# Block products in the last two thirds of an MLP's first layer, and attention tiles moved forward to feed them

## The reference

```python
# q, k, v: [4, 8, 576, 64], chunks of 64 tokens
scores = (q_c @ k_c.T) / 8;  attn = softmax(scores);  out = attn @ v_c
x = out as [2304 tokens, 512]
h = x @ w_in;  g = h - tanh(h);  x = g @ w_out                      # MLP 1, w_in [512, 2048]
h = x @ w2_in; g = h * tanh(softplus(h));  out = g @ w2_out         # MLP 2
```

## Time and profile before

| | |
|---|---|
| median of the runs | 824.29 us |
| time of the profiled execution | 823.91 us |
| its span, first to last instruction | 822.1 us |
| TensorE busy (matmul) | 812.8 us, 99% |
| VectorE busy | 543.9 us, 66% |
| ScalarE busy | 361.9 us, 44% |
| GpSimd busy | 150.5 us, 18% |
| DMA traffic | 132.21 MB, mean 161 GB/s |

### The profile page before, as it was taken

One profiled execution on the slowest core, in us unless ns is written; L12 is line 12 of the kernel. 1 busy time (PEld: TensorE's weight loads), 2 busy tenths in 40 slices (PEclk: granted clock), 3 DMA queues, 4 the chain that ended last, 5 costly groups with the idle time before them and its releaser, 6 DMA issues.

```text
span 822.1 us, 13517 instructions
## 1 busy us (share of the span) xinstructions
PE 812.8 (99%) x5394; PEld 765.6 (93%) x5394; DVE 543.9 (66%) x819; ACT 361.9 (44%) x567; POOL 150.5 (18%) x213
## 2 busy tenths in 40 slices
PE   7999999999999999999999999999999999999998
PEld 6999999999999999999999889888988988888896
DVE  6766555655555655534447788888877777877775
ACT  4544433343344344333335455546445435445434
POOL 4322244334415413410110111110000000000000
PEclk9999999999999999999999999999999999999999
DMA  7653355444425434422654265397424276523302
GB/s 242 210 177 99 101 186 193 133 159 180 168 74 198 157 115 157 179 65 90 231 194 164 90 231 192 129 354 311 153 92 177 90 272 236 195 90 127 143 0 77
DMA packets 41597, 132.21 MB, mean 161 GB/s; under 512 B 7104, under 2 KB 10944, under 8 KB 41536
## 3 DMA queue, kind: packets, MB, share of 16 engines
q1 hardware_dynamic: 29088, 83.38, 28.2%
q0 software_dynamic: 12448, 47.98, 16.6%
HBM read 91.49 MB, written 35.91 MB: 155 GB/s over the span
## 4 chain that ended last, share of the span: by engine, by line
PE 91%; DVE 5%; ACT 2%; issue 1%; DMA 0%; SPq 0%
PE psum L945 8%; PE psum L946 8%; PE psum L944 8%; PE psum L931 8%; PE psum L932 7%; PE psum L933 7%; PE psum L1080 7%; PE psum L1081 7%; PE psum L1079 7%; PE psum L1058 6%; PE psum L1059 6%; PE psum L1057 6%; PE psum L892 1%; PE psum L858 1%; PE psum L978 1%
## 5 line engine op out<-in xcount | busy, mean ns | idle before, releaser
L673 DVE TENSOR_TENSOR pool_words<-psum,pool_words 128x384 f32<-128x384 f32 x96 | 53.4, 557 | 120.3 <-ACT pool_words L466 120.3
L946 PE MATMUL psum<-g_hi,w_lo 128*128 128x384 f32 x384 | 128.4, 334 | 0.0
L945 PE MATMUL psum<-g_lo,w_hi 128*128 128x384 f32 x384 | 128.3, 334 | 0.0
L944 PE MATMUL psum<-g_hi,w_hi 128*128 128x384 f32 x384 | 128.3, 334 | 0.0
L931 PE MATMUL psum<-x_hi,w_hi 128*128 128x384 f32 x360 | 122.2, 340 | 0.7 <-DVE w_lo L606 0.7
L932 PE MATMUL psum<-x_lo,w_hi 128*128 128x384 f32 x360 | 120.4, 334 | 0.0
L933 PE MATMUL psum<-x_hi,w_lo 128*128 128x384 f32 x360 | 120.3, 334 | 0.0
L466 ACT ACTIVATE pool_words<-psum 128x384 f32<-128x384 f32 x96 | 46.9, 489 | 146.3 <-PE psum L933 144.3
L1058 PE MATMUL psum<-w_lo,w_hi 128*128 128x384 f32 x288 | 97.5, 339 | 0.0
L1059 PE MATMUL psum<-w_hi,w_lo 128*128 128x384 f32 x288 | 97.0, 337 | 0.0
L1057 PE MATMUL psum<-w_hi 128*128 128x384 f32 x288 | 96.3, 334 | 0.0
(11 more groups left out here) (110 smaller groups left out, 1532.1 us busy)
## 6 DMA issues: line engine op xcount, KB each, us to landing
w_hi<-s_hi SPq DMA_DIRECT2D x24, 896.0 KB, 4.6
w_lo<-s_lo SPq DMA_DIRECT2D x24, 896.0 KB, 6.8
pool_words<-w_out POOLq DMA_DIRECT2D x32, 256.0 KB, 3.8
w_hi<-t_hi SPq DMA_DIRECT2D x18, 384.0 KB, 4.9
w_lo<-t_lo SPq DMA_DIRECT2D x18, 384.0 KB, 5.6
pool_words<-w POOLq DMA_DIRECT2D x24, 256.0 KB, 3.7
pool_words<-qT SPq DMA_DIRECT2D x18, 256.0 KB, 3.8
pool_words<-kT SPq DMA_DIRECT2D x18, 256.0 KB, 5.1
```

The costliest lines, as they stand in the source:

```text
L944: pe.matmul(ps, w_hi[:, 1, cols], g_hi[:, s, :], start=f == 0, stop=False)
L945: pe.matmul(ps, w_hi[:, 1, cols], g_lo[:, s, :], start=False, stop=False)
L946: mm = pe.matmul(ps, w_lo[:, 1, cols], g_hi[:, s, :], start=False, stop=f == FT - 1)
```

## The change

Groups 0 and 1 of MLP 1 stay plain (`PLAIN = 2`). The other four groups become two supers of 768 tokens, done as MLP 2 is: 16 pairs q = 0 to 15 of seven block products (`product1`, six matmuls of 128x384), six additions each, then tanh, subtraction and the two parts on 768 columns. `y1_wide(u, j)`, the output step, keeps the weights stationary as `y1` does and takes 768 tokens as three matmuls of 512 and three of 256. Eight more sets of weight sums are made (now of `w_in` too), stored and loaded back. The second super's input sums are made in place, without a way through HBM.

The input of the first super is tiles 6 to 11, so all attention tiles up to 11 must be finished in groups 0 and 1: nine blocks stand there instead of six. The other six stand behind the products of pairs 0 to 5 (tiles 12 to 17). The bodies of `order_blocks`, `turn_blocks`, `shift`, `normalise`, `wait_for_values`, `scores`, `values`, `hidden` and `y1` are unchanged, and so is the order within an f of `mlp1_group`. The buffers in `pool_words` are laid out anew.

```diff
+PLAIN = 2
...
+ORDER1 = (M1, M2, M6, M7, M4, M5, M3)
...
+BLOCK_AT = {(0, 5): 3, (0, 8): 4, (0, 11): 5, (0, 14): 6, (1, 1): 7, (1, 4): 8, (1, 7): 9, (1, 9): 10, (1, 11): 11}
+BLOCK_BEHIND = {0: 12, 2: 13, 3: 14, 4: 15, 5: 16, 6: 17}
+STEPS_AFTER = {1: (0, 0, 0, 0, 1, 1, 2), PAIRS + 1: (2, 2, 0, 0, 1, 1, 2)}
+STEPS_BESIDE_PAIR = (2, 0, 2, 0, 2, 1, 1)
+STEPS_BESIDE_BLOCK = (1, 1, 0, 0, 1, 1, 1)
...
+place_steps([("group", 0, f) for f in (12, 13, 14)], weight_steps(0))
+place_steps([("group", 1, f) for f in range(1, 13)], [step for j in range(1, 5) for step in weight_steps(j)])
+place_steps([(1, 1), (1, 2), (1, 3)], _T0[0:3])
+place_steps([(2, 1), (2, 2), (2, 3)], [_T0[3], weight_steps(5)[0], _T0[4]])
+place_steps([(3, 1), (3, 2), (3, 3)], [weight_steps(5)[1], _T0[5], weight_steps(5)[2]])
+place_steps([(4, 0), (4, 1), (4, 2), (4, 3)], [_T0[6]] + weight_steps(6))
+place_steps([(5, 1), (5, 2), (5, 3)], weight_steps(7))
+place_steps([(6, 1), (6, 2), (6, 3)], weight_steps(8))
+place_steps([(PAIRS, 3), (PAIRS + 1, 1), (PAIRS + 1, 2), (PAIRS + 1, 3)], weight_steps(9)[0:2] + [_T1[0], weight_steps(9)[2]])
+for _i in range(1, 7):
+    place_steps([(PAIRS + 1 + _i, r) for r in range(4)], [_T1[_i]] + weight_steps(9 + _i))
+EARLY_STEPS = len(STEPS)
...
+            def add_x(w):
+                b11, b21, b12, b22 = (x_block(w, t, k) for t in range(2) for k in (0, HALF_K))
+                pool.wait_ge(x_next_done, (9, 15)[w])
+                pool.tensor_tensor(b12, b22, b12, ALU.subtract).then_inc(x_sums, 1)
+                pool.wait_ge(x1_lo_done, 7 * w + 1)
+                pool.wait_ge(x_sums, 4 * w + 1)
+                pool.tensor_tensor(b11, b12, b11, ALU.add).then_inc(x_sums, 1)
+                pool.wait_ge(x1_lo_done, 7 * w + 2)
+                pool.wait_ge(x_sums, 4 * w + 2)
+                pool.tensor_tensor(b21, b11, b21, ALU.subtract).then_inc(x_sums, 1)
+                pool.wait_ge(x1_lo_done, 7 * w + 3)
+                pool.wait_ge(x_sums, 4 * w + 3)
+                pool.tensor_tensor(b11, b22, b11, ALU.subtract).then_inc(x_sums, 1)
+            def load_w2_out(v):
+                if v >= 2:
...
+            for t in range(GROUP_TILES, 13):
                 sp.wait_ge(scores_ready, t)
                 load_qk(t)
                 if t > GROUP_TILES:
                     order_blocks(t - 1)
                 sp.wait_ge(values_ready, t)
                 load_v(t)
-            order_blocks(TILES - 1)
-            before = FT * (GROUPS - 1)
-            for pair in range(2):
-                sp.wait_ge(h_ready, before - (-(pair + 1) * 7 * BLOCK // D_MODEL))
-                load_slot(pair)
-            for i in range(7):
-                end = FT if i == M3 else -(-(2 * 7 * BLOCK + (i + 1) * WIDE) // D_MODEL)
-                sp.wait_ge(h_ready, before + end)
-                load_tokens(0, i)
+                if t in (10, 11):
+                    sp.wait_ge(h_ready, FT - (-(t - 9) * 7 * BLOCK // D_MODEL))
+                    load_slot(t - 10)
+            sp.wait_ge(scores_ready, 13)
+            load_qk(13)
+            order_blocks(12)
+            for q in range(PAIRS1):
+                if q == PAIRS1 - 1:
+                    for i in range(7):
+                        sp.wait_ge(product1_ready, 7 * q + i + 1)
+                        load_tokens(0, i)
+                sp.wait_ge(product1_ready, 7 * (q + 1))
+                if q not in BLOCK_BEHIND:
+                    load_slot(q + 2)
+                    continue
+                t = BLOCK_BEHIND[q]
+                sp.wait_ge(values_ready, t + 1)
+                if t + 1 < TILES:
+                    load_v(t + 1)
+                if t + 2 < TILES:
+                    sp.wait_ge(scores_ready, t + 2)
+                    load_qk(t + 2)
+                load_slot(q + 2)
+                if t + 1 < TILES:
+                    order_blocks(t + 1)
...
+            def mlp1_pair(q):
+                if q - 1 in BLOCK_BEHIND and BLOCK_BEHIND[q - 1] + 1 < TILES:
+                    exps(BLOCK_BEHIND[q - 1] + 1)
+                beside_pair_hi(q, 0)
+                keep_m1_1(q)
+                if q == 0:
+                    split_g_hi(PLAIN * FT - 1)
+                    x1_hi(0, 6)
+                if q == 1:
+                    keep_y(1)
+                if q > 0:
+                    hi1(2 * q - 1)
+                beside_pair_hi(q, "w0")
+                if q == PAIRS + 1:
+                    keep_wide_y(0)
+                for r in range(1, 4):
+                    beside_pair_hi(q, r)
+                beside_pair_hi(q, "w1")
+                tanh1(2 * q)
+                hi1(2 * q)
+                tanh1(2 * q + 1)
+                if q in BLOCK_BEHIND:
+                    keep_x(BLOCK_BEHIND[q])
 
             exps(0)
             exps(1)
@@ -534,8 +755,11 @@
...
+            def mlp1_pair(q):
+                scored = BLOCK_BEHIND.get(q - 1, TILES) + 1
+                if scored < TILES:
+                    shift(scored)
+                if q > 0:
+                    minus1(2 * q - 1)
+                beside_pair_lo(q, 0)
+                if q > 0:
+                    lo1(2 * q - 1)
+                take1_c11(q)
+                if q == 0:
+                    split_g_lo(PLAIN * FT - 1)
+                beside_pair_lo(q, "w0")
+                if q == 1:
+                    keep_y(1)
+                take1_u2(q)
+                if q == 0:
+                    x1_lo(0, 6)
+                if scored < TILES:
+                    normalise(scored)
+                beside_pair_lo(q, 1)
+                take1_u3(q)
+                if scored < TILES:
+                    turn_blocks(scored)
+                if q == PAIRS + 1:
+                    keep_wide_y(0)
+                beside_pair_lo(q, 2)
+                take1_c21(q)
+                beside_pair_lo(q, 3)
+                take1_c22(q)
+                beside_pair_lo(q, "w1")
+                minus1(2 * q)
+                take1_c12(q)
+                lo1(2 * q)
 
             shift(0)
             shift(1)
@@ -734,8 +1064,11 @@
             split_chunk_lo(1)
             split_chunk_lo(2)
             minus_tanh(0)
...
+            def product1(q, place):
+                w, r, i = q // PAIRS, q % 2, ORDER1[place]
+                pe.wait_ge(slot_loaded[r], 32 * (q // 2 + 1))
+                if q % PAIRS == 0:
+                    pe.wait_ge(x1_lo_done, 7 * w + place + 1)
...
+                    pe.wait_ge(x_next_done, t - 2)
+                    if t + 1 < TILES:
+                        pe.wait_ge(shifted, t + 2)
+                if q == 0 and place in (2, 3):
+                    pe.wait_ge(g_done, PLAIN * FT - 3 + place)
+                if q == 1 and place < 4:
+                    pe.wait_ge(sums1_taken, (2, 3, 4, 6)[place])
+                if q > 1 and place < 2:
+                    pe.wait_ge(sums1_taken, 6 * (q - 1) + (4, 6)[place])
+                if q > 1 and place == 2 or q == 0 and place == 4:
+                    pe.wait_ge(m1_kept1, q + 1)
+                if q > 1 and place == 3 or q == 0 and place == 5:
+                    pe.wait_ge(sums1_taken, 6 * q + 1)
+                if q > 0 and place in (4, 5):
+                    pe.wait_ge(sums1_taken, 6 * q + place - 2)
+                if place == 6:
+                    pe.wait_ge(sums1_taken, 6 * q + 5)
+                ps = product1_ps(q, place)
+                t_hi_words = token_words(w_hi, x_hi, place).rearrange("p (k n) -> p k n", k=HALF_K)
+                t_lo_words = token_words(w_lo, x_lo, place).rearrange("p (k n) -> p k n", k=HALF_K)
+                for k in range(HALF_K):
+                    first, end = i != M3 and k == 0, i != M5 and k == HALF_K - 1
...
+            def y1_wide(u, j):
+                w, f = u // (UNITS1 // 2), unit_tile(u)
+                start, end = u % (UNITS1 // 2) == 0, u % (UNITS1 // 2) == UNITS1 // 2 - 1
...
+                    pe.wait_ge(lo1_done, u + 1)
+                    if u == 0:
+                        pe.wait_ge(m1_kept1, 2)
+                        pe.wait_ge(sums1_taken, 6 + 1)
+                    if start:
+                        pe.wait_ge(y_kept, (2 * KT, 2 * KT + 6)[w])
+                at = slice(f * D_MODEL + j * P, f * D_MODEL + (j + 1) * P)
+                u_hi, u_lo = unit_words(g_hi, x_hi, u), unit_words(g_lo, x_lo, u)
+                half_bank = bank[4 + j // 2][:, j % 2 * 256:j % 2 * 256 + 256]
+                pe.matmul(bank[j], w_hi[:, 1, at], u_hi[:, 0:512], start=start, stop=False)
+                pe.matmul(bank[j], w_hi[:, 1, at], u_lo[:, 0:512], start=False, stop=False)
+                pe.matmul(bank[j], w_lo[:, 1, at], u_hi[:, 0:512], start=False, stop=end)
+                pe.matmul(half_bank, w_hi[:, 1, at], u_hi[:, 512:WIDE], start=start and j % 2 == 0, stop=False, skip_group_check=True)
+                pe.matmul(half_bank, w_hi[:, 1, at], u_lo[:, 512:WIDE], start=False, stop=False, skip_group_check=True)
```

(52 more changed lines are left out.)

646 lines of the change are left out of this document (395 added, 251 removed).

## The result

| | before | after |
|---|---|---|
| median | 824.28 us (6 runs) | 1032.14 us (6 runs, 1027.09 to 1036.55) |
| time and span of the profiled execution | 823.91, 822.1 us | 1034.47, 1032.7 us |
| TensorE busy | 812.8 us, 99% | 856.5 us, 83% |
| DMA traffic | 132.21 MB | 180.48 MB |

The ratio is 1.2521, with a 95% interval of 1.2482 to 1.2559. The forecast was 874.8 us with a range of 847 to 896: the sign is right, the size is not. The change costs 207.9 us and not 50.5.

What follows compares the result with a forecast made beforehand. The prediction took TensorE, busy 99% of the span, to bound the kernel; -13.8 (matmul work) + 32.8 (blocks in groups) + 4 (clock) + 25 (blocks behind pairs) + 2.5 (seams) = +50.5 us, a median of 874.8 us, range 847 to 896.

Steps and rivals of the forecast that it cites:

- part 3: Pairs 0 to 5 with blocks behind them: VectorE's order makes them too long, +25 us (5 to 35); pairs without blocks nothing.
- part 4: Seams in pair 9 and MLP 2's pair 1: +2.5 us (0 to 6); added stores and loads cost nothing.
- a stored step: Sign that the forecast is wrong: a stall released by a stored step, which it costed at nothing.
- Part 1: TensorE's matmul work: hidden and y1 removed in four groups, block products and output steps added, -13.8 us (-16.9 to +7.4).
- rival (c): Output steps: weight loads hold the 256-column matmuls at 0.173 us, +21 on the forecast, 896 us; chance 0.07.
- Part 2: Nine blocks in groups 0 and 1: TensorE waits for ordered blocks, +32.8 us (25 to 40).
- the clock (+4): Groups 0 and 1: TensorE may lose its clock in three waits of 6.5 us, +4 us, between nothing and 10.
- the walk: Groups 0 and 1: 12.7 us from the scores' end to ordered blocks, 16 us from tile to tile.
- (a): Groups 0 and 1 and pairs: the blocks don't wait, so the kernel is faster, 813 us; chance 0.05.
- (f): Whole kernel: small waits eat the gain and no more, near 824 us; chance 0.05.
- (b): Blocks wait in groups 0 and 1, but VectorE's order in the pairs is covered by 5 us: 853 us; chance 0.2.
- (d): Clock lost in each long wait and in the pairs as well: +6 to +15, about 885 us; chance 0.13.

Runs made afterwards that it cites:

- e2: Kernel after, without all steps beside the pairs (weight sets 5 to 15, token parts of the first two supers), so output isn't the reference's: 902.14 us.
- e5: Kernel after, with one more 512-column buffer for the steps of groups 0 and 1: 1018.44 us.
- e8: Kernel before, with the attention blocks of groups 1 to 4 three steps of f apart (f = 8, 11, 14 instead of 4, 9, 14): 854.91 us.
- e12: Kernel after, with extra step buffers, stores ahead of additions, ScalarE issuing half the order transfers, blocks behind y1 and early normalise and turn: 932.05 us.
- e9: Kernel after, with the attention block of groups 0 and 1, and its wait, moved behind the y1 matmuls: 1001.64 us.

## Why the prediction was right in sign and wrong in size

**The step that failed** is in part 3 and part 4: "In the ten pairs without a block VectorE has ... 12 of 15.7 us, and each addition comes before the product that needs its bank: nothing", and "the added stores and loads ... lie a pair ahead of their use ...: nothing; if late, some us a pair". The first counts VectorE's busy time but not what a step waits for. The second looks at when the stored blocks are used, and not at when the buffer that they are stored from comes free. The runs put 130 us on the steps beside the pairs (e2), of which one more buffer in pairs 8 to 15 gives 32 back and the order of GpSimd's work 33 (59 together, about nine tenths of it in the pairs). That much is shown to be the wait for a buffer whose store hasn't landed; the rest of the 130 is shown to come with the steps, but not by which of their waits. The waits for "a stored step" stood in the forecast only as a sign that would make it wrong, without a price. The price was to be had from the kernel before: four additions of 0.83 us ahead of a step's store, and the landing (in the median 3.4 us after its issue for the high half of a token part, 4.6 for the low one), against four steps in a pair of 15.7 us.

**Part 1 (-13.8) and part 4's seams (+2.5) hold as far as the runs show.** 256-column matmuls start 0.116 us apart in the mean, against the 0.118 taken; rival (c) is dead. One output step of the dense pair 8 shows them:

```profile
436.29 0.39 PE L1358 MATMUL psum<-g_hi,w_lo 128*128 128x512 f32 x1
436.52 0.28 PE L1360 MATMUL psum<-g_hi,w_hi 128*128 128x256 f32 x1
436.63 0.28 PE L1361 MATMUL psum<-g_lo,w_hi 128*128 128x256 f32 x1
436.75 0.28 PE L1362 MATMUL psum<-g_hi,w_lo 128*128 128x256 f32 x1
436.87 0.34 PE L1337 MATMUL psum<-w_hi 128*128 128x384 f32 x1
```

The figure of the Trainium skill (TensorE: Matmul & The Clock Gate, Back-to-back issue gap), as an estimate 0.109 us by its 262 cycles, is 6% short here. Without steps, pair 9 is 17.45 us against 15.7, the 1.7 forecast for its seam; in MLP 2 e2 has 1.7 us more than its work explains, where 0.8 was forecast.

**Part 3's blocks (+25): right in kind.** They stand behind pairs 0 and 2 to 6 (`BLOCK_BEHIND`); the text ahead of the result says "pairs 0 to 5", which is a slip, though it left the count of six. Without steps pairs 2 to 6 exceed their work of 17.1 us by 0, 3.8, 2.6, 6.1 and 4.2, pair 0 by 0.5, and pair 1 its 11.6 by 2.4, not by 7.5: 19.6 us in all. That is from below, as e2 takes VectorE's steps away as well, so that pairs 3 to 6 come out as walked is in part luck. For all of the kernel but groups 0 and 1, the forecast is -13.8 + 25 + 2.5, less the three blocks moved out (3.9), plus the two `y1` moved in (4.2): 14.0. In e2, 276.9 - 273.3 = 3.6 in the pairs and 6.0 in MLP 2 make 9.6.

**Part 2 (+32.8) and the clock (+4) were too small.** With the three blocks moved in (3.9) and the two `y1` moved out (4.2) they make 36.5; measured are 69.2. TensorE's waits are 43.4 for the blocks and 6.5 once for the input split. That last one is the step buffer again (e5): "GpSimd's steps lie at f = 1 to 12, one set per three f, and fit" had no wait for a store in it. With the same work on both sides that leaves 19.6 us (73.4 - 3.9 - 43.4 - 6.5), and the work at half clock is worth 19. The cycles are longer than the walk for two reasons. First, the chain: behind tile 7's block, which starts at 127.4 and ends at 128.9, SyncE's first issue comes 6.4 us later, as in the earlier trace rows. But the eight issues take 5.32 us and not 4.96, and y1 resumes at 144.4, 4.4 us after the last was issued, where the earlier trace rows has 1.9. That is 15.5 us and not 12.7. Of the chains ahead of tiles 4 to 11, all but that of tile 7 (where the input split comes between), one takes 12.7 us, the other six 13.8 to 16.0, nearly all of the difference in the last landing. The median of the earlier trace rows hid this: in the kernel before, too, single landings take up to 4.1 us. Second, y1 behind the wait runs at half clock, and a cycle is 15.5 + 4.1 + 1.4 = 21 us where I had 16; four of eight measured cycles are 20.3 to 21.1. The forecast gave the clock a price for the three longest waits only; in e8 it is also lost at four of eight waits, of 2.6 to 4.0 us. The rule on the clock, which the forecast cites from the Trainium skill (TensorE: Matmul & The Clock Gate, What's actually happening), had the better direction: its 10 us is nearer to 19 than the 4 taken.

**Rivals.** (a) and (f) are refuted by the result. (b) had the pairs' chain covered but for 5 us; e2 has 19.6 even with VectorE's steps away. (d), clock lost in the pairs too, was right as an effect (0.83 and 0.86 there, worth 34 us) but most of it follows from waits that no rival had. None of them, and no part of the range, held a wait of ScalarE for a store.

**Open.** What holds the remaining 70.8 us of e12 in the pairs was not separated: two `y1` moved in (4.2), ScalarE's waits for GpSimd's weight additions, the stores that still share a buffer in pairs 1 to 6, and half clock (worth 24 us there) are all in it. No run kept the steps and took every wait for a store away, nor gave GpSimd's additions to another engine. A version with block products in the last super alone, which would leave the blocks their old distances, was not tried, nor were stores issued by SyncE.

## What to carry to other kernels

When a change lays out memory anew, list for each staging buffer how long it is held: produced, queued behind the storing engine's other work, stored, landed. Set that time against the distance to the next producer. A buffer too few doesn't show in busy time; it shows as a wait in front of a cheap instruction, and all that stands behind that instruction in its engine's order inherits it. Price a wait on TensorE as its length plus, unless the traces show otherwise, the work behind it at half clock (e8 has both cases), and put what can run ahead of a wait ahead of it (e9, 30 us for a move of two lines). When a wait hangs on the last of several transfers, price its landing by the slow ones in the trace, and not by the median.

## What the runs showed of the hardware

- **The clock falls after some short waits, and late.** In e8 it stays full behind four waits of 2.1 to 2.3 us; behind three of 2.6 to 4.0 us TensorE resumes at full clock and goes to half clock in the middle of the work. In the kernel after, a wait of 2.2 us (ahead of tile 6) has the same effect. The kernel after is at half clock for 184 us, e9 for 141, e12 for 89, the kernel before for 1.
- **Small transfers land later in the kernel after.** The 32 KB order transfers, same code and same size, take a median of 2.7 us there against 1.9. The kernel after moves more data, but that this is the reason wasn't tested: in e8, with the traffic and the median of the kernel before, y1 still resumes 3.5 and 3.8 us after the last issue at two of its waits, and 1.9 and 2.0 at two others.

```profile
pool_words<-pool_words SPq DMA_DIRECT2D x120, 32.0 KB, 2.7
```

- **A store of 384 KB is not short.** The low half of a token part lands 5.5 us (median) after its issue, the high half, issued 0.5 us earlier, after 3.5. For weight parts of the same size it is 3.5 and 2.7.
